# Adding the residual inside the mixing products' bank by TensorE transposes, instead of by kept copies and VectorE additions

## The chip, the cores and the metric

One core of a Trainium2 chip runs the whole program. The metric is the device time of one execution in microseconds (us). The kernel before takes 549.34 us (median of 3 runs, 549.34 to 549.35).

## The reference, cut to what matters

The program computes sparse attention, then a layer norm with a two-layer MLP (`x + relu(xn @ w_ch1) @ w_ch2`), and then a mixing block. The change is in the last one:

```
theta = x @ w_theta                           # x: (2, 768, 512)
zr, zi = x * cos(theta), x * sin(theta)
y = einsum('ts,bsd->btd', w_tok_r, zr) + einsum('ts,bsd->btd', w_tok_i, zi)
u = x + y
out = u + relu(u @ w_ch)
```

All values are float32. The products run on pairs: a value is split into a high part and a rest (`hi`, `lo`), and three products (hi*hi, hi*lo, lo*hi) stand for one.

## The kernel before, in words

The four working engines and SP each run their own list of instructions, written out in order; semaphores tie them together. Tokens are cut into 12 tiles of 128 (2 batches of 6), the 512 channels into 4 blocks of 128. `x` holds a token tile with tokens on partitions. The mixing wants its result the other way, channels on partitions (`y` transposed), so that the channel product can follow.

**Rotation.** For each token tile t (12 of them), `rotation_tensor` (L1313) first runs the 12 theta products of tile t-1 (L1323: 3 for each of 4 channel blocks, 512 columns) and then transposes tile t's four 128x128 blocks into `x2T_bank` (L1333). `rotation_scalar` (L1256) copies this bank to `x2Th` (L1261), then copies it a second time into a home that lasts (L1268, `x2T_home`, signal `x2T_kept`): two tiles have homes of their own, the others take the x tile of two tiles earlier, once its rotation is done (wait on `z_ready`). Then it computes abs and two sines for tile t-1 (L1276, L1277, L1279) and the high part of z for tile t-2 (L1284). `rotation_vector` (L1287) reduces theta to a fraction of a turn in three steps (L1295, L1297, L1299), subtracts for `x2Tl` (L1303), and makes `z_lo` (L1309). TensorE's next transposes wait for `x2T_split` and `x2T_kept`. GpSimd multiplies x by cosine and sine (L1232) and splits the token weights: SP loads a tile (L1190), GpSimd writes its high part (L1212) and its rest (L1215) into a ring of three slots, signal `tok_split`. A slot is free again once `ring_used` is raised, or, for the last tile of a group, once `y_mm` is. The last quarter of the MLP (L1087, L1105) runs between the first seven rotation steps.

**Mixing.** There are four groups n, one for each batch b and half th of the output tokens (384 columns). `mix(n)` in `mixing_tensor` runs over 6 input tiles s and 4 channel blocks d, with 6 products of 384 columns each (L1471), 144 in a group; each d has a PSUM bank of its own. In group 0, rotation steps 7 to 12 stand between its tiles. With the last s, each d raises `y_mm`. Then `u_add` (L1398) on VectorE adds the kept transposed x to the bank, in 3 pieces of 128 columns, into `u_sum`; ScalarE copies that to `uTh` (L1395); `u_low` subtracts for `uTl` (L1414). `channels(n)` (L1479) multiplies u by `w_ch` into the same banks (48 products, L1489), and runs one group late: the order on TensorE is mix 0, mix 1, channels 0, mix 2, channels 1, mix 3, channels 2, channels 3. `outputs(n)` on VectorE (L1424, L1428) forms u + relu, and SP stores it.

Of the kernel before, what the change touches and what calls it, by code (L numbers as in the profile page):

```python
# [20 lines left out]
F32 = mybir.dt.float32  # L21
# [66 lines left out]
def program(nc, qT, kcols, vwin, kT, v, limits, g_ln, w1, w2, w_theta, wtokT, w_ch, outT):  # L88
    with ExitStack() as ctx:
# [1053 lines left out]
        out_sb = placed("out_sb", 56, [P, 2, CN])  # L1143
        u_sum = placed("u_sum", 59, [P, 2, CN])

# [8 lines left out]
        c_hi, ch_hi, theta_split, ch_split, tok_split = sem("c_hi"), sem("ch_hi"), sem("theta_split"), sem("ch_split"), sem("tok_split")  # L1154
        x2T_mm, x2T_hi, x2T_split, x2T_kept = sem("x2T_mm"), sem("x2T_hi"), sem("x2T_split"), sem("x2T_kept")
        theta_mm, round_step, frac_ready, trig_ready = sem("theta_mm"), sem("round_step"), sem("frac_ready"), sem("trig_ready")
        abs_ready = sem("abs_ready")
        z_ready, z_high, z_split = sem("z_ready"), sem("z_high"), sem("z_split")
        ring_used, y_mm, u_added, u_high, u_split = sem("ring_used"), sem("y_mm"), sem("u_added"), sem("u_high"), sem("u_split")
        v_mm, u_summed, out_ready = sem("v_mm"), sem("u_summed"), sem("out_ready")  # L1160
        out_stored = [sem(f"out_stored{s}") for s in range(2)]

        MIX = [(b, th) for b in range(BATCH) for th in range(HALVES)]

        x2T_second = placed("x2T_second", 30, [P, DC, P])

        def x2T_home(t):

            if t == 0:
                return raw[:, 0, :, :].rearrange("p c n -> p (c n)")[:, DC * (FQ - P):].rearrange(  # L1170
                    "p (c n) -> p c n", c=DC)
            if t == 1:
                return x2T_second[:, :, :]
            return x_tile((t - AT) // TILES, (t - AT) % TILES)

# [32 lines left out]
        def mixing_pool(pool):  # L1208
# [8 lines left out]
            def split_tok(j):  # L1217
                pool.wait_ge(tok_loaded[j % 2], 16 * (j // 2 + 1))
                if j >= RING:
                    n, used = divmod(j - RING, TILES)  # L1220
                    if used == TILES - 1:
                        pool.wait_ge(y_mm, (n + 1) * DC)
                    else:
                        pool.wait_ge(ring_used, n * (TILES - 1) + used + 1)
                split(ring_h[j % RING][:, :, :], ring_l[j % RING][:, :, :], raw_tok[:, j % 2, :, :], tok_split)
# [30 lines left out]
        def rotation_scalar(act, t):  # L1256
            if t < TT:
                act.wait_ge(x2T_mm, t + 1)
                if t >= 2:
                    act.wait_ge(theta_mm, t - 1)  # L1260
                nc.scalar.activation(x2Th[:, t % 2, :, :].rearrange("p c n -> p (c n)"), x2T_bank[:, :],  # L1261
                                     ACT.Copy).then_inc(x2T_hi, 1)
                if t == 0:
                    act.wait_ge(theta_split, 1)
                elif t >= AT:
                    act.wait_ge(z_ready, t - AT + 1)
                act.wait_ge(x2T_split, t + 1)
                nc.scalar.activation(x2T_home(t), x2T_bank[:, :].rearrange("p (c n) -> p c n", c=DC),  # L1268
                                     ACT.Copy).then_inc(x2T_kept, 1)
            if 1 <= t < TT + 1:  # L1270
                m = t - 1
                s = m % 2
                act.wait_ge(frac_ready, m + 1)
                if m >= 2:
                    act.wait_ge(z_split, m - 1)
                nc.scalar.activation(frac[:, s, 1, :], frac[:, s, 0, :], ACT.Abs).then_inc(abs_ready, 1)  # L1276
                nc.scalar.activation(trig[:, s, 1, :], frac[:, s, 0, :], ACT.Sin, scale=TWO_PI)  # L1277
                act.wait_ge(abs_ready, m + 1)
                nc.scalar.activation(trig[:, s, 0, :], frac[:, s, 1, :], ACT.Sin, scale=-TWO_PI,  # L1279
                                     bias=half_pi[:, 0:1]).then_inc(trig_ready, 1)  # L1280
            if 2 <= t < TT + 2:
                m = t - 2
                act.wait_ge(z_ready, m + 1)
                nc.scalar.activation(z_hi[m // TILES][:, m % TILES, :, :], trig[:, m % 2, :, :],  # L1284
                                     ACT.Copy).then_inc(z_high, 1)
# [27 lines left out]
        def rotation_tensor(pe, t):  # L1313
# [12 lines left out]
            if t < TT:  # L1326

                pe.wait_ge(ch_added, CT * CHUNKS * LATE + t + 1)
                if t >= 1:
                    pe.wait_ge(x2T_split, t)  # L1330
                    pe.wait_ge(x2T_kept, t)
                for d in range(DC):
# [50 lines left out]
        def mixing_scalar(act):  # L1383
# [5 lines left out]
            for k in range(len(MIX) * DC):  # L1389
                th, d = MIX[k // DC][1], k % DC  # L1390
                act.wait_ge(u_added, CT * (k + 1))
                if k >= HALVES * DC:

                    act.wait_ge(out_ready, k - HALVES * DC + DC - d)
                nc.scalar.activation(uTh[:, th, d, :], u_sum[:, k % 2, :], ACT.Copy).then_inc(u_high, 1)  # L1395

        def mixing_vector(dve):
            def u_add(n, d):  # L1398

                b, th = MIX[n]  # L1400
                k = n * DC + d
                if k >= 2:
                    dve.wait_ge(u_split, k - 1)
                dve.wait_ge(y_mm, k + 1)
                for i in range(CT):
                    cols = slice(i * P, (i + 1) * P)
                    nc.vector.tensor_tensor(u_sum[:, k % 2, cols], mix_bank[th][d][:, cols],
                                            x2T_home(b * TILES + th * CT + i)[:, d, :], ALU.add).then_inc(u_added, 1)

            def u_low(n, d):  # L1410

                th, k = MIX[n][1], n * DC + d
                dve.wait_ge(u_high, k + 1)
                nc.vector.tensor_tensor(uTl[:, th, d, :], u_sum[:, k % 2, :],  # L1414
                                        uTh[:, th, d, :].bitcast(F32), ALU.subtract).then_inc(u_split, 1)

# [19 lines left out]
            for n in range(len(MIX)):  # L1436
                for d in range(DC + 1):
                    if d < DC:
                        u_add(n, d)
                    if d >= 1:  # L1440
                        u_low(n, d - 1)
                if n >= 1:
# [3 lines left out]
        def mixing_tensor(pe):  # L1446
            def mix(n):

                b, th = MIX[n]
                for s in range(TILES):  # L1450
# [5 lines left out]
                    for d in range(DC):  # L1456
# [7 lines left out]
                        if s == 0 and n == 1 and d == 0:  # L1464
                            pe.wait_ge(frac_ready, TT)
                            pe.wait_ge(x2T_kept, TT)
                        if s == 0 and n >= 2:
                            pe.wait_ge(out_ready, (n - 2) * DC + d + 1)
                        for r in range(2):
                            for m, (zt, wt) in enumerate(((z_hi, ring_h), (z_hi, ring_l), (z_lo, ring_h))):  # L1470
                                last = nc.tensor.matmul(bank, zt[b][:, s, r, ds], wt[j % RING][:, r, :],  # L1471
                                                        start=(s == 0 and r == 0 and m == 0),
                                                        stop=(s == TILES - 1 and r == 1 and m == 2))
                        if s == TILES - 1:
                            last.then_inc(y_mm, 1)
                    if s < TILES - 1:
# [88 lines left out]
```

## Time and profile before

| | |
|---|---|
| time, median of 3 | 549.34 us |
| profiled execution: its own time, and its span | 549.34 us, 547.5 us |
| PE (TensorE products) busy | 537.8 us (98%) |
| PEld (TensorE weight loads) busy | 482.0 us (88%) |
| DVE (VectorE) busy | 266.2 us (49%) |
| ACT (ScalarE) busy | 171.2 us (31%) |
| POOL (GpSimd) busy | 185.7 us (34%) |
| granted TensorE clock, mean | 1.00 |

Busy time is the union of an engine's instructions. Products overlap in the pipeline, so the record of a 384-column product is about twice as long as the distance from its start to the next one's: for a rate, starts are compared and not durations. The rotation runs from about 347 us on, the mixing from about 395 us to the end.

### The profile page before, as it was taken

The page shows a single profiled execution, that of the slowest core. Times are in us where ns is not written, and L with a number is a line of the kernel's source. Part 1 is how long each engine was busy: PE and PEld are TensorE (multiplying, and loading weights), DVE is VectorE, ACT ScalarE, POOL GpSimd, SP SyncE. Part 2 cuts the span into 40 slices and gives each one's busy share as a digit, 9 for nine tenths or more (in the row PEclk, how much of TensorE's full clock was granted, in tenths as well). Part 3 has the DMA queues.
Part 4 walks back from the last instruction along what each step waited for, and adds up shares of the span by engine and source line. Part 5 has one row for each costly group of instructions (what it writes and reads, how often), then busy time and mean ns, then how long its engine had stood idle before and what let it go on. Part 6 is the DMA issues. An engine that isn't in the chain of part 4 may idle for free.

```text
span 547.5 us, 8685 instructions
## 1 busy us (share of the span) xinstructions
PE 537.8 (98%) x3376; PEld 482.0 (88%) x3376; DVE 266.2 (49%) x678; ACT 171.2 (31%) x438; POOL 185.7 (34%) x165
## 2 busy tenths in 40 slices
PE   8899999999999999999999999999999999999997
PEld 7788788788888888998889998888799999999997
DVE  7765655556547454222222322355865669307054
ACT  5564443444435332111111111265555422001010
POOL 6596000000000000398000410033499799362500
PEclk9999999999999999999999999999999999999999
DMA  7663243211221000033100110000022133341202
GB/s 227 199 221 90 83 146 113 74 56 45 87 65 45 1 1 2 0 135 101 73 1 0 54 34 1 0 1 1 1 57 63 55 86 88 115 116 62 83 21 95
DMA packets 24810, 36.95 MB, mean 67 GB/s; under 512 B 2240, under 2 KB 17600, under 8 KB 24768
## 3 DMA queue, kind: packets, MB, share of 16 engines
q1 hardware_dynamic: 24768, 36.38, 21.4%
q8 instruction: 27, 0.44, 0.3%
q14 instruction: 15, 0.12, 0.1%
HBM read 33.23 MB, written 3.15 MB: 66 GB/s over the span
## 4 chain that ended last, share of the span: by engine, by line
PE 81%; POOL 10%; DVE 4%; issue 3%; ACT 1%; DMA 0%; POOLq 0%; DVEq 0%; ACTq 0%
PE bank L882 13%; PE bank L865 13%; PE bank L1471 12%; PE bank L1087 12%; PE bank L1105 11%; PE bank L1489 6%; POOL trig L1232 4%; PE bank L535 4%; PE bank L505 3%; PE bank L520 3%; POOL ring_l L1215 3%; PE bank L1323 3%; POOL ring_h L1212 2%; POOL bias L412 1%; PE bank L803 1%
## 5 line engine op out<-in xcount | busy, mean ns | idle before, releaser
L865 PE MATMUL bank<-xnT,w1h 128*128 128x256 f32 x384 | 73.7, 291 | 1.3 <-DVE xnT L826 1.3
L865 PEld LDWEIGHTS bank<-xnT,w1h 128*128 128x128 f32 x384 | 59.7, 191 | 7.2 <-issue 5.0
L1087 PE MATMUL bank<-xnT,w1h 128*128 128x384 f32 x256 | 65.2, 335 | 0.0
L1471 PE MATMUL bank<-ring_h,z_hi 128*128 128x384 f32 x192 | 65.0, 338 | 0.1
L1471 PE MATMUL bank<-ring_h,z_lo 128*128 128x384 f32 x192 | 64.3, 335 | 0.0
L1471 PE MATMUL bank<-ring_l,z_hi 128*128 128x384 f32 x192 | 64.2, 335 | 0.0
L484 ACT ACTIVATE sp_buf<-sp_buf,row_max 128x256 f32<-128x256 f32 (+1 forms) x96 | 46.0, 481 | 42.3 <-DVE row_max L428 42.3
L795 POOL TENSOR_TENSOR rstd<-rtmp,minus_half 128x2 f32<-128x2 f32 x6 | 4.2, 697 | 154.6 <-DVE rtmp L766 154.6
L1232 POOL TENSOR_TENSOR trig<-x,trig 128x512 f32<-128x512 f32 x24 | 32.8, 1387 | 67.7 <-ACT trig L1279 67.7
L865 PE MATMUL bank<-xnT,w1l 128*128 128x256 f32 x192 | 54.3, 283 | 0.0
L1215 POOL TENSOR_TENSOR ring_l<-raw,ring_h 128x768 fp32r<-128x768 f32 x24 | 48.0, 2001 | 2.0
L1087 PEld LDWEIGHTS bank<-xnT,w1h 128*128 128x128 f32 x256 | 46.4, 188 | 0.6
L1068 ACT ACTIVATE hTh<-bank 128x384 fp32r<-128x384 f32 x32 | 15.5, 490 | 99.4 <-PE bank L1087 99.4
L1087 PE MATMUL bank<-xnT,w1l 128*128 128x384 f32 x128 | 42.9, 335 | 0.0
L882 PE MATMUL bank<-w2h,hTh 128*128 128x512 f32 x96 | 40.8, 425 | 1.6 <-DVE hTl L845 1.3
L1048 DVE SCALAR_TENSOR_TENSOR hTl<-bank,hTh 128x384 fp32r<-128x384 f32 x32 | 17.7, 557 | 50.6 <-ACT hTh L1068 50.6
L1105 PE MATMUL bank<-w2h,hTh 128*128 128x512 f32 x96 | 38.0, 396 | 0.0
L882 PE MATMUL bank<-w2h,hTl 128*128 128x512 f32 x96 | 37.7, 393 | 0.0
L882 PE MATMUL bank<-w2l,hTh 128*128 128x512 f32 x96 | 37.7, 393 | 0.0
L1105 PE MATMUL bank<-w2h,hTl 128*128 128x512 f32 x96 | 37.6, 392 | 0.0
L428 DVE CUSTOM_DVE_ANT_0 sp_buf<-bank,bias 128x256 f32<-128x256 f32 (+1 forms) x96 | 32.9, 398 | 9.7 <-PE bank L505 7.7
L1105 PE MATMUL bank<-w2l,hTh 128*128 128x512 f32 x96 | 37.5, 391 | 0.0
(124 smaller groups left out, 1124.9 us busy)
## 6 DMA issues: line engine op xcount, KB each, us to landing
raw<-wtokT SPq DMA_DIRECT2D x24, 384.0 KB, 3.2
raw<-w SPq DMA_DIRECT2D x8, 1024.0 KB, 5.7
v_sb<-vwin SPq DMA_DIRECT2D x16, 256.0 KB, 2.7
k_sb<-kcols SPq DMA_DIRECT2D x16, 200.0 KB, 3.3
q_sb<-qT SPq DMA_DIRECT2D x24, 128.0 KB, 2.8
outT<-out_sb SPq DMA_DIRECT2D x16, 192.0 KB, 1.8
v_sb<-vwin SPq DMA_DIRECT2D x8, 192.0 KB, 2.9
k_sb<-kcols SPq DMA_DIRECT2D x8, 136.0 KB, 2.8
```

The source lines that it names most:

```text
L428: nc.vector.tensor_tensor_reduce(out=sp_buf[:, k % 2, u, h, 0:w], in0=score_banks(k)[h][:, u * WIN:u * WIN + w], in1=table_of[:, 2 * hp + ...
L484: nc.scalar.activation(scores, scores, ACT.Exp, scale=-1.0, bias=row_max[:, AT * k + u, h:h + 1], accum_out=den[:, AT * (k % DENS) + u, h, ...
L535: last = nc.tensor.matmul(o_bank(k)[DH * h:DH * (h + 1), u * P:(u + 1) * P], v_sb[:, s, value_chunk(t, u, c), DH * h:DH * (h + 1)], probsT ...
L865: last = nc.tensor.matmul(bank_of(n)[:, 0:AN], wt[q][:, d, f * P:(f + 1) * P], xnT[:, AT * c:AT * c + AT, low, d, :], start=(d == 0 and m ...
L882: last = nc.tensor.matmul(bank_of(n)[:, :], ht[:, f, i * P:(i + 1) * P], wt[q][:, f, :], start=(f == 0 and m == 0), stop=(f == FC - 1 and ...
L1048: nc.vector.scalar_tensor_tensor(hTl[:, f, :], h_bank[f % 2][:, 0:CN], 0.0, hTh[:, f, :].bitcast(F32), ALU.max, ALU.subtract).then_inc(h_s ...
L1087: last = nc.tensor.matmul(h_bank[f % 2][:, 0:CN], wt[slot][:, d, fs], tokens(low, d), start=first, stop=(d == DC - 1 and wt is w1l))
L1105: last = nc.tensor.matmul(ch_bank[i][:, :], ht[:, f, ts], wt[slot][:, f, :], start=(f == 0 and n == 0), stop=(f == FC - 1 and n == 2))
L1215: nc.gpsimd.tensor_tensor(lo, src, hi.bitcast(F32), ALU.subtract).then_inc(done, 1)
L1232: last = nc.gpsimd.tensor_tensor(tr, x_tile(t // TILES, t % TILES), tr, ALU.mult)
L1471: last = nc.tensor.matmul(bank, zt[b][:, s, r, ds], wt[j % RING][:, r, :], start=(s == 0 and r == 0 and m == 0), stop=(s == TILES - 1 and ...
L1489: last = nc.tensor.matmul(mix_bank[th][e][:, 0:CN], wt[:, d, es], ut[:, th, d, :], start=(d == 0 and m == 0), stop=(d == DC - 1 and m == 2))
```

## The change: the diff

The kept copies, their homes, `u_sum` and the additions go. When the last product of a bank in a mixing group is issued, three transposes (`is_transpose=True`, `start=False`) of the x blocks of those output tokens follow into the three 128-column pieces of the same bank; `y_mm` is raised behind the last one. ScalarE's `uTh` copy and VectorE's `uTl` subtraction read the bank. `ring_used` is now raised for each of a group's six tiles, for the sixth ahead of the last bank's transposes, and the ring's waits use it throughout.

```diff
--- before.py
+++ after.py
@@ -1141,7 +1141,6 @@
         ring_h = [placed(f"ring_h{s}", kb, [P, 2, CN], F32R) for s, kb in enumerate((24, 112, 118))]
         ring_l = [placed(f"ring_l{s}", kb + 3, [P, 2, CN], F32R) for s, kb in enumerate((24, 112, 118))]
         out_sb = placed("out_sb", 56, [P, 2, CN])
-        u_sum = placed("u_sum", 59, [P, 2, CN])
 
         x2T_bank, theta_bank = banks[0], (banks[1], banks[7])
         mix_bank = [banks[2:6], [banks[6], banks[7], banks[0], banks[1]]]
@@ -1152,26 +1151,15 @@
         theta_loaded, ch_loaded = sem("theta_loaded"), sem("ch_loaded")
         tok_loaded = [sem(f"tok_loaded{s}") for s in range(2)]
         c_hi, ch_hi, theta_split, ch_split, tok_split = sem("c_hi"), sem("ch_hi"), sem("theta_split"), sem("ch_split"), sem("tok_split")
-        x2T_mm, x2T_hi, x2T_split, x2T_kept = sem("x2T_mm"), sem("x2T_hi"), sem("x2T_split"), sem("x2T_kept")
+        x2T_mm, x2T_hi, x2T_split = sem("x2T_mm"), sem("x2T_hi"), sem("x2T_split")
         theta_mm, round_step, frac_ready, trig_ready = sem("theta_mm"), sem("round_step"), sem("frac_ready"), sem("trig_ready")
         abs_ready = sem("abs_ready")
         z_ready, z_high, z_split = sem("z_ready"), sem("z_high"), sem("z_split")
-        ring_used, y_mm, u_added, u_high, u_split = sem("ring_used"), sem("y_mm"), sem("u_added"), sem("u_high"), sem("u_split")
+        ring_used, y_mm, u_high, u_split = sem("ring_used"), sem("y_mm"), sem("u_high"), sem("u_split")
         v_mm, u_summed, out_ready = sem("v_mm"), sem("u_summed"), sem("out_ready")
         out_stored = [sem(f"out_stored{s}") for s in range(2)]
 
         MIX = [(b, th) for b in range(BATCH) for th in range(HALVES)]
-
-        x2T_second = placed("x2T_second", 30, [P, DC, P])
-
-        def x2T_home(t):
-
-            if t == 0:
-                return raw[:, 0, :, :].rearrange("p c n -> p (c n)")[:, DC * (FQ - P):].rearrange(
-                    "p (c n) -> p c n", c=DC)
-            if t == 1:
-                return x2T_second[:, :, :]
-            return x_tile((t - AT) // TILES, (t - AT) % TILES)
 
         def x_block(b, q, i):
             return x_tiles[:, b, i // AT, q, i % AT, :]
@@ -1217,11 +1205,7 @@
             def split_tok(j):
                 pool.wait_ge(tok_loaded[j % 2], 16 * (j // 2 + 1))
                 if j >= RING:
-                    n, used = divmod(j - RING, TILES)
-                    if used == TILES - 1:
-                        pool.wait_ge(y_mm, (n + 1) * DC)
-                    else:
-                        pool.wait_ge(ring_used, n * (TILES - 1) + used + 1)
+                    pool.wait_ge(ring_used, j - RING + 1)
                 split(ring_h[j % RING][:, :, :], ring_l[j % RING][:, :, :], raw_tok[:, j % 2, :, :], tok_split)
 
             def rotate(t):
@@ -1260,13 +1244,6 @@
                     act.wait_ge(theta_mm, t - 1)
                 nc.scalar.activation(x2Th[:, t % 2, :, :].rearrange("p c n -> p (c n)"), x2T_bank[:, :],
                                      ACT.Copy).then_inc(x2T_hi, 1)
-                if t == 0:
-                    act.wait_ge(theta_split, 1)
-                elif t >= AT:
-                    act.wait_ge(z_ready, t - AT + 1)
-                act.wait_ge(x2T_split, t + 1)
-                nc.scalar.activation(x2T_home(t), x2T_bank[:, :].rearrange("p (c n) -> p c n", c=DC),
-                                     ACT.Copy).then_inc(x2T_kept, 1)
             if 1 <= t < TT + 1:
                 m = t - 1
                 s = m % 2
@@ -1328,7 +1305,6 @@
                 pe.wait_ge(ch_added, CT * CHUNKS * LATE + t + 1)
                 if t >= 1:
                     pe.wait_ge(x2T_split, t)
-                    pe.wait_ge(x2T_kept, t)
                 for d in range(DC):
                     last = nc.tensor.transpose(x2T_bank[:, d * P:(d + 1) * P], x_block(t // TILES, d, t % TILES),
                                                ident[:, :])
@@ -1388,31 +1364,19 @@
             nc.scalar.activation(wch[:, :, :], raw_ch, ACT.Copy).then_inc(ch_hi, 1)
             for k in range(len(MIX) * DC):
                 th, d = MIX[k // DC][1], k % DC
-                act.wait_ge(u_added, CT * (k + 1))
+                act.wait_ge(y_mm, k + 1)
                 if k >= HALVES * DC:
 
                     act.wait_ge(out_ready, k - HALVES * DC + DC - d)
-                nc.scalar.activation(uTh[:, th, d, :], u_sum[:, k % 2, :], ACT.Copy).then_inc(u_high, 1)
+                nc.scalar.activation(uTh[:, th, d, :], mix_bank[th][d][:, 0:CN], ACT.Copy).then_inc(u_high, 1)
 
         def mixing_vector(dve):
-            def u_add(n, d):
-
-                b, th = MIX[n]
-                k = n * DC + d
-                if k >= 2:
-                    dve.wait_ge(u_split, k - 1)
-                dve.wait_ge(y_mm, k + 1)
-                for i in range(CT):
-                    cols = slice(i * P, (i + 1) * P)
-                    nc.vector.tensor_tensor(u_sum[:, k % 2, cols], mix_bank[th][d][:, cols],
-                                            x2T_home(b * TILES + th * CT + i)[:, d, :], ALU.add).then_inc(u_added, 1)
-
-            def u_low(n, d):
-
-                th, k = MIX[n][1], n * DC + d
-                dve.wait_ge(u_high, k + 1)
-                nc.vector.tensor_tensor(uTl[:, th, d, :], u_sum[:, k % 2, :],
-                                        uTh[:, th, d, :].bitcast(F32), ALU.subtract).then_inc(u_split, 1)
+            def u_low(n):
+                th = MIX[n][1]
+                for d in range(DC):
+                    dve.wait_ge(u_high, n * DC + d + 1)
+                    nc.vector.tensor_tensor(uTl[:, th, d, :], mix_bank[th][d][:, 0:CN],
+                                            uTh[:, th, d, :].bitcast(F32), ALU.subtract).then_inc(u_split, 1)
 
             def outputs(n):
                 th = MIX[n][1]
@@ -1434,11 +1398,7 @@
             nc.vector.tensor_tensor(wcl[:, :, :], raw_ch, wch[:, :, :].bitcast(F32),
                                     ALU.subtract).then_inc(ch_split, 1)
             for n in range(len(MIX)):
-                for d in range(DC + 1):
-                    if d < DC:
-                        u_add(n, d)
-                    if d >= 1:
-                        u_low(n, d - 1)
+                u_low(n)
                 if n >= 1:
                     outputs(n - 1)
             outputs(len(MIX) - 1)
@@ -1463,15 +1423,19 @@
                                 pe.wait_ge(ch_added, CT * CHUNKS * LATES - CT + d - 1)
                         if s == 0 and n == 1 and d == 0:
                             pe.wait_ge(frac_ready, TT)
-                            pe.wait_ge(x2T_kept, TT)
                         if s == 0 and n >= 2:
                             pe.wait_ge(out_ready, (n - 2) * DC + d + 1)
                         for r in range(2):
                             for m, (zt, wt) in enumerate(((z_hi, ring_h), (z_hi, ring_l), (z_lo, ring_h))):
                                 last = nc.tensor.matmul(bank, zt[b][:, s, r, ds], wt[j % RING][:, r, :],
-                                                        start=(s == 0 and r == 0 and m == 0),
-                                                        stop=(s == TILES - 1 and r == 1 and m == 2))
+                                                        start=(s == 0 and r == 0 and m == 0), stop=False)
                         if s == TILES - 1:
+                            if d == DC - 1:
+                                last.then_inc(ring_used, 1)
+                            for i in range(CT):
+                                last = nc.tensor.matmul(bank[:, i * P:(i + 1) * P], x_block(b, d, th * CT + i),
+                                                        ident[:, :], start=False, stop=(i == CT - 1),
+                                                        is_transpose=True)
                             last.then_inc(y_mm, 1)
                     if s < TILES - 1:
                         last.then_inc(ring_used, 1)
```

## Rows read from the trace of the kernel before

**Rows 1.** The page, the chain that ended last, by engine

```profile
PE 81%; POOL 10%; DVE 4%; issue 3%; ACT 1%; DMA 0%; POOLq 0%; DVEq 0%; ACTq 0%
```

**Rows 2.** Chain of waits, pieces from 442 us: start us, us, what

```profile
442.37 1.85 POOL ring_l L1215
...
444.26 17.08 PE bank L1471 x96
...
502.94 24.96 PE bank L1471 x144
527.90 16.66 PE bank L1489 x96
```

**Rows 3.** Busy by stretch: length, PE, PEld, DVE, ACT, POOL, clock, DMA share, GB/s

```profile
347.00:391.70 44.70, 43.79 (x215) 36.70 (x214) 24.13 (x36) 22.90 (x38) 13.08 (x10) 1.00 0.00 1
391.70:444.30 52.60, 52.46 (x285) 48.86 (x285) 34.43 (x35) 26.28 (x40) 45.56 (x31) 1.00 0.19 53
444.30:545.00 100.70, 100.25 (x576) 99.74 (x576) 46.39 (x98) 10.33 (x17) 45.52 (x30) 1.00 0.27 85
```

**Rows 4.** Instruction groups of PE, 391.7 to 443.8: busy, mean ns, idle

```profile
L1471 PE MATMUL bank<-ring_h,z_hi 128*128 128x384 f32 x64 | 21.9, 342 | 0.0
...
L1323 PE MATMUL bank<-wth,x2Tl 128*128 128x512 f32 x24 | 9.5, 394 | 0.0
...
L1333 PE MATMUL bank<-ident,x 128*128 128x128 f32 x20 | 3.0, 273 | 0.0
```

**Rows 5.** One line's instructions (L1333), then PE's timeline: start, us, what

```profile
L1333 PE MATMUL bank<-ident,x x48: 272/273/273, 347.6 to 424.4; 128*128 128x128 f32 x48
...
424.07 0.60 PE L1333 MATMUL bank<-ident,x 128*128 128x128 f32 x4
424.43 0.42 PE L1471 MATMUL bank<-ring_h,z_hi 128*128 128x384 f32 x1
424.69 0.33 PE L1471 MATMUL bank<-ring_l,z_hi 128*128 128x384 f32 x1
```

**Rows 6.** PE's timeline, earlier short products, and line L505's records

```profile
23.78 0.95 PE L893 MATMUL bank<-ident 128*128 128x128 f32 x7
...
41.80 1.04 PE L520 MATMUL bank<-ident,sp_buf 128*128 128x128 f32 x8
...
60.44 1.14 PE L535 MATMUL bank<-probsT,v_sb 128*64 128x128 f32 x16
...
L505 PE MATMUL bank<-k_sb,q_sb x192: 271/377/632, 4.8 to 191.0; 64*128 64x256 f32 x160, 64*128 64x128 f32 x32
```

**Rows 7.** The kept copy, L1268: its records, and who waited (no line follows)

```profile
L1268 ACT ACTIVATE x<-bank x10: 597/599/602, 362.3 to 427.3; 128x512 f32<-128x512 f32 x10
...
who waited for it (us, times):
```

**Rows 8.** PE's timeline at one theta step, and ahead of 444 us

```profile
384.92 0.40 PE L1105 MATMUL bank<-w2h,hTl 128*128 128x512 f32 x1
385.74 0.47 PE L1323 MATMUL bank<-wth,x2Th 128*128 128x512 f32 x1 [0.42 <-DVE x2Tl L1303]
...
443.79 0.34 PE L1471 MATMUL bank<-ring_h,z_lo 128*128 128x384 f32 x1
```

**Rows 9.** Timelines of DVE and POOL

```profile
384.91 0.68 DVE L1303 TENSOR_TENSOR x2Tl<-bank,x2Th 128x512 fp32r<-128x512 f32 x1
...
394.63 2.73 POOL L1232 TENSOR_TENSOR trig<-x,trig 128x512 f32<-128x512 f32 x2 [3.25 <-ACT trig L1279]
...
431.55 2.73 POOL L1232 TENSOR_TENSOR trig<-x,trig 128x512 f32<-128x512 f32 x2 [3.02 <-ACT trig L1279]
```

**Rows 10.** Instruction groups, 372 to 548 us: busy, mean ns, idle before

```profile
L1414 DVE TENSOR_TENSOR uTl<-u_sum,uTh 128x384 fp32r<-128x384 f32 x16 | 14.5, 918 | 0.3
...
L1407 DVE TENSOR_TENSOR u_sum<-bank,x 128x128 f32<-128x128 f32 x40 | 9.4, 284 | 42.2 <-PE bank L1471 42.0
L1395 ACT ACTIVATE uTh<-u_sum 128x384 fp32r<-128x384 f32 x16 | 8.4, 526 | 73.9 <-DVE u_sum L1407 73.8
```

## The prediction

> **What bounds the kernel now.** I read the chain of waits first: 81% of it is TensorE, 10% GpSimd [rows 1]. The change touches the last third of the program, so I followed that chain from 442 us: at 444.26 it leaves GpSimd's ring split for TensorE, and from there to 544.56 it is nothing but L1471 and L1489, back to back, with one DVE add and the store behind them [rows 2]. Then the busy times by stretch: after 444.3 TensorE is busy 100.25 of 100.70 us, and its weight loads 99.74, at clock 1.00; DVE, ACT and GpSimd have half or more of the stretch free. From 391.7 to 444.3 TensorE has 52.46 of 52.60 us, and before it 43.79 of 44.70 [rows 3].
>
> Modelled busy time can hide waiting, and the chain between 388 and 444 us runs over GpSimd, so I checked the second stretch by start-to-start distances. L1471 takes 24.96 us for 144 products, 0.173 us each [rows 2]. L1323 has 512 columns instead of 384 and starts every 0.23 us (0.173 x 512/384 = 0.231, my estimate); a transpose starts every 0.11 us, as shown below. The stretch from 391.70 to 443.8 holds 3 x 64 products of L1471, 3 x 24 of L1323 and 20 transposes [rows 4]: 192 x 0.173 + 72 x 0.23 + 20 x 0.11 = 33.2 + 16.6 + 2.2 = 52.0 us of the 52.3 that passed. So TensorE really runs without a gap there too, and GpSimd keeps pace beside it. The bound is TensorE's instruction count from about 391 us to the end.
>
> **What the change adds on TensorE.** For each of 4 (batch, half) groups and 4 banks, three transposes of 128 columns are put in front of the y_mm signal: 4 x 4 x 3 = 48. Their x block is the loaded weight and ident streams, as in L1333, of which the trace has 48 records for the 12 x 4 that the code issues, so one record each [rows 5]. The price by L1333: a group of four starts at 424.07 and has 0.60 us from first start to last end, the last lasting 0.273, so three distances in 0.327 us, 0.109 each; and the second product behind it starts at 424.69, where without the group it would have started at 424.07 + 0.173: 0.62 - 0.173 = 0.447 us for four, 0.112 each, the switch to fp32 and back included [rows 5]. Eight of L520 give the same 0.109 ((1.04 - 0.275)/7) [rows 6]. A 128-column stream costs that much although 384 columns take 0.173: each transpose needs its own weights, and the next load starts only as the previous stream begins. The load ahead of the first transpose hides under the product before it, the load for the product behind the last one does not, so I take three as 3 x 0.11. Sum: 48 x 0.11 = 5.28 us.
>
> Bounds for one such accumulating transpose, which the trace does not show (all the ones it has overwrite their columns): from below L535, 128 columns with a half-wide weight, (1.14 - 0.28)/15 = 0.057 us, 2.7 us in all; from above an ordinary fp32 product, which leaves two records (L505: 192 for the 24 x 4 that the code issues), and whose records start every (0.95 - 0.275)/6 = 0.1125 us at L893 [rows 6]: 0.225 us, 10.8 us in all. I take L1333's 0.11: it is the same instruction on the same operands apart from the accumulate flag, and products in this trace that accumulate go at the rate of their columns.
>
> The trace's price for a lone stream can be set against the Trainium skill, "TensorE: Matmul & The Clock Gate", section "Back-to-back issue gap", which gives about 81 ns per load-and-product pair at 128 columns once sustained. By that figure the 48 would be an estimated 3.9 us. The trace's rows give 0.109 to 0.112, and I stay with them.
>
> All 48 are in program order on TensorE. The 12 at the end of the first mixing group fall at about 435.6 us, the other 36 in the stretch that the chain follows to the end. No engine's slack covers them, with one exception. At 443.79 the last product ahead of the ninth ring tile starts and the next at 444.26, 0.47 instead of 0.173 us [rows 8, 2]: TensorE waits 0.30 us for GpSimd's ring_l, which ends at 444.22. The first 12 transposes bring TensorE there 1.32 us later, and GpSimd does not move (its split waits on a ring slot freed before the transposes). So that 0.30 us goes: 5.28 - 0.30 = **+4.98 us**. What is late next is TensorE itself. If GpSimd were also 1.3 us later there, the 0.30 would stay: +5.28.
>
> **What the change takes from DVE and ACT in the mixing.** 48 additions of 0.28 us on DVE (40, 4 and 4 in three groups) go; the ACT copy and the DVE subtraction stay and read a bank instead of u_sum [rows 10]. Worth nothing: ACT sat idle 73.8 us for these copies, and the products that want u_split start a whole mixing group later, except in the last group, where the 8.3 us of channels(2) (half of the 16.66 at 527.90 [rows 2]) stand before channels(3). The banks are held until the subtraction ends, which channels(n) waited for before. If reading the bank made the subtraction slower (0.918 us mean now [rows 10]), even 2 us for each of the four would just fill those 8.3 us. The last add and the store are unchanged.
>
> **What it takes from the rotation.** 12 ACT copies of 0.60 us go, with the waits before them and TensorE's x2T_kept wait; nobody in the trace waited for these copies, TensorE included [rows 7]. What ACT sat idle ahead of them it sits idle later, at abs, for z_lo. The two real stalls of TensorE there are another's: theta's first product starts at 385.74, 0.82 us after the product before instead of 0.23 (0.59 lost; 0.62 again at 391.70), released by x2Tl [rows 8]. x2Tl runs at 384.91, right behind DVE's own three frac steps, which start when the previous theta ends [rows 9]; no ACT copy stands in that chain. Value taken: 0. The end above: ACT's relief somehow removes both, -1.21. The end below: earlier sines let GpSimd rotate beside DVE more often and delay x2Tl once more, +0.6. The re-aimed ring waits (ring_used for y_mm) free a slot at the same product as before: 0.
>
> **Sum.** Against the profiled execution's own 549.34 us (span 547.5 and 1.84 around it): 549.34 + 4.98 = **554.3 us**. The median of the three runs is the same 549.34, so nothing is to be shifted. +0.91%.
>
> **Rivals.**
> (a) Cheaper transposes or freed stalls: 48 x 0.057 = 2.7 less 0.3 gives 551.8; price 0.11 with both theta stalls gone gives 549.34 + 4.98 - 1.21 = 553.1. For it: only one of the three loads needs to hide. Against: two families of transposes at 0.109. Chance 0.09.
> (b) The accumulating transpose does not get the short form and runs as an ordinary fp32 product, so the change doesn't do what it says: 48 x 0.225 - 0.3 = +10.5, 559.8 us. For it: no such instruction is in the trace. Against: the same transpose flag as L1333's. Chance 0.07.
> (c) Not slower: GpSimd, not TensorE, paces 388 to 444 us, as the chain says. Then what it waited for ACT's sines counts, 3.25 us at 394.63 and 3.02 at 431.55 [rows 9], and with ACT rid of its copies and of the z_ready wait these 6.27 us come back, with the 0.30: 5.28 - 6.57 = -1.3, 548.0 us. It decides from the point at which TensorE's 52.3 us hold more than 5 us of waiting. Against it: my count leaves 0.3 us. Chance 0.03, with 0.01 for stopping within 0.2%.
> (d) The granted clock falls to 1.2 GHz over the new groups. In the rows it is 1.00 over all twelve groups of L1333 [rows 3]. Half rate over a bank's last six products and its three transposes (6 x 0.173 + 0.33 = 1.37 us) would add 1.37 us, 16 times: 549.34 + 4.98 + 21.9 = 576 us. Chance 0.01.
> What (d) goes by is the same page of the Trainium skill, section "Part 4: PE-mode transpose", which says that transposes do not count as activity for the clock gate. The trace shows no fall behind groups of four or eight, so it bears the rule out at no place that matters here.
>
> **Chances.** Forecast 0.79; (a) 0.09, (b) 0.07, (c) 0.04, (d) 0.01. Range 552.2 to 556.0: below, most of (a); above, the missing 0.30, the 0.6 of a new stall and 0.01 us more for each transpose. Outside are (b), (c), (d) and the bottom of (a), some 0.15. A difference under 0.2% (1.1 us) can't be told from none here. Faster 0.03, same 0.01, slower 0.96.
>
> **What would show it.** The new transpose line: 48 records, starts 0.11 us apart; 0.22 and 96 records mean (b). Each mixing group from 444 us on 1.3 us longer, 26.3 instead of 24.96; channels still 8.32. The wait for ring_l at the ninth tile gone; theta's stalls still two, released by x2Tl. Clock 1.00 throughout. DVE's and ACT's busy time down by about 14 and 7 us, with no effect on the end. The forecast is wrong if the mixing groups keep 24.96 us, or if 391 to 444 us shrinks by more than 1 us.

## The result, and the profile after

The changed kernel takes 554.49 us (median of 4 runs, 554.33 to 554.70), the kernel before 549.34 us beside it: ratio 1.0094, interval 1.0077 to 1.0112. It is slower, by 5.15 us. The forecast was 554.3 us and +0.91%. The profiled execution took 554.20 us, 4.86 more than the profiled one of before; the sum of the prediction said 4.98.

The page of the changed kernel, its shares of the chain (compare [rows 1]):

```profile
PE 92%; DVE 4%; POOL 1%; issue 1%; ACT 1%; DMA 0%; DVEq 0%; POOLq 0%; ACTq 0%
```

GpSimd's 10% are down to 1%. GpSimd did not get faster: TensorE's wait for it at 444 us is gone, and with it the way by which the chain used to step over to GpSimd's list for 55 us. A share of the chain says where the walk back went, and 0.3 us of waiting can decide that.

The chain of waits from 471 us to the end (start us, us, what; compare [rows 2]):

```profile
471.80 21.85 PE bank L1430 x126
493.65 0.33 PE bank L1436 x3
493.98 1.05 PE bank L1430 x6
...
497.79 0.33 PE bank L1436 x3
498.12 8.33 PE bank L1453 x48
506.44 21.85 PE bank L1430 x126
...
532.76 16.66 PE bank L1453 x96
```

L1430 is the mixing product (L1471 before), L1436 the new transpose, L1453 the channel product (L1489 before). A mixing group runs from 471.80 to 498.12, 26.32 us instead of 24.96; the channel products keep 8.33 and 16.66.

Busy times by stretch, columns as in [rows 3], up to the last rotation product, then up to the first, second and third block of channel products:

```profile
391.72:431.48 39.76, 39.76 (x213) 36.48 (x213) 27.02 (x29) 17.96 (x29) 32.98 (x22) 1.00 0.22 60
431.48:463.23 31.75, 31.75 (x193) 31.45 (x192) 14.77 (x14) 9.67 (x15) 28.79 (x18) 1.00 0.26 75
463.23:497.87 34.64, 34.64 (x207) 34.49 (x206) 7.84 (x12) 1.97 (x4) 16.10 (x12) 1.00 0.30 92
497.87:532.51 34.64, 34.64 (x207) 34.49 (x206) 7.85 (x12) 1.97 (x4) 10.71 (x8) 1.00 0.18 57
```

TensorE is busy all of each, at clock 1.00. The first stretch took 39.76 us before as well, with ACT busy 21.54 instead of 17.96: the missing copies show on ACT and nowhere in time. Two rows for it and the second stretch, of the kernel before:

```profile
391.70:431.46 39.76, 39.76 (x213) 36.47 (x213) 26.98 (x29) 21.54 (x35) 32.98 (x22) 1.00 0.21 60
431.46:461.18 29.72, 29.58 (x169) 29.08 (x168) 21.08 (x34) 9.81 (x14) 28.37 (x17) 1.00 0.26 72
```

The second one grew by 2.03 us, with 24 transposes in it; the third and fourth, 33.28 us each before (by the chain, 24.96 + 8.32), by 1.36 us with 12 each.

The new line's records, and TensorE's timeline around the first group of three (compare [rows 5]):

```profile
L1436 PE MATMUL bank<-ident,x x48: 270/272/273, 432.5 to 532.5; 128*128 128x128 f32 x48
```

```profile
432.36 0.34 PE L1430 MATMUL bank<-ring_h,z_lo 128*128 128x384 f32 x1
432.54 0.49 PE L1436 MATMUL bank<-ident,x 128*128 128x128 f32 x3
432.78 0.42 PE L1430 MATMUL bank<-ring_h,z_hi 128*128 128x384 f32 x1
433.04 0.34 PE L1430 MATMUL bank<-ring_l,z_hi 128*128 128x384 f32 x1
```

48 records, so the short form. From 432.36 to 433.04 there are 0.68 us, 0.35 of them for the two long products: 0.33 for three transposes. Three starts span 0.49 - 0.272 = 0.218 us, 0.109 apart, and the rest falls on the next product, which is followed after 0.26 us instead of 0.173.

### The profile page after: what moved, and what is told of

It is laid out like the page before. It is cut to its first block, busy times and chain, and to the rows that moved or that the text cites. A ratio compares the mean times of both kernels' runs of the same rounds, so it can differ in the third digit from the quotient of the medians.

```text
span 552.4 us, 8695 instructions
## 1 busy us (share of the span) xinstructions
PE 542.3 (98%) x3424; PEld 486.5 (88%) x3424; DVE 250.4 (45%) x630; ACT 163.7 (30%) x426; POOL 183.2 (33%) x165
## 4 chain that ended last, share of the span: by engine, by line
PE 92%; DVE 4%; POOL 1%; issue 1%; ACT 1%; DMA 0%; DVEq 0%; POOLq 0%; ACTq 0%
PE bank L1430 18%; PE bank L882 13%; PE bank L865 13%; PE bank L1087 12%; PE bank L1105 11%; PE bank L1300 6%; PE bank L1453 6%; PE bank L535 4%; PE bank L505 3%; PE bank L520 3%; POOL bias L412 1%; PE bank L1436 1%; PE bank L1309 1%; PE bank L803 1%; PE bank L545 1%
## 5 line engine op out<-in xcount | busy, mean ns | idle before, releaser
L1430 PE MATMUL bank<-ring_h,z_hi 128*128 128x384 f32 x192 | 65.9, 343 | 0.0
L1430 PE MATMUL bank<-ring_h,z_lo 128*128 128x384 f32 x192 | 64.4, 336 | 0.0
L1430 PE MATMUL bank<-ring_l,z_hi 128*128 128x384 f32 x192 | 64.3, 335 | 0.0
L1203 POOL TENSOR_TENSOR ring_l<-raw,ring_h 128x768 fp32r<-128x768 f32 x24 | 46.8, 1951 | 2.0
L1200 POOL TENSOR_SCALAR ring_h<-raw 128x768 fp32r<-128x768 f32 x24 | 25.2, 1050 | 36.9 <-DMA raw<-wtokT 25.3
```

The source lines that it names most:

```text
L1200: nc.gpsimd.tensor_scalar(hi, src, 1.0, 0.0, ALU.mult, ALU.add).then_inc(c_hi, 1)
L1203: nc.gpsimd.tensor_tensor(lo, src, hi.bitcast(F32), ALU.subtract).then_inc(done, 1)
```

## The experiments

The edits are cut to the lines that matter. In e1, e3, e4 and e6 the ring's waits are also those of the kernel before.

The theory under test: TensorE's list is the bound, each transpose costs 0.11 us wherever it stands, what left DVE and ACT was free, and the one thing gained is the wait for the ninth ring tile (`ring_l`, the rest of a token weight tile that GpSimd splits).

**e1: the removals alone.** The 48 transposes are left out, so the residual is not added.

```diff
-                            for i in range(CT):
-                                last = nc.tensor.matmul(bank[:, i * P:(i + 1) * P], x_block(...), ident[:, :], ...)
                             last.then_inc(y_mm, 1)
```

> The changed kernel with its 48 transposes left out, so the residual is not added to u; the ring waits are those of before. All that the change removes is gone, and what it adds too. Theory (the removed copies and additions are worth nothing, TensorE's instruction count is the bound): 549.3 us, with the wait for ring_l at the ninth tile back. Rival (the relief of ACT, DVE or GpSimd is worth something, and the transposes cost more than 5.1 us): 548.1 us or less.

Measured: 549.41 us (median of 10, 549.29 at best), ratio to before 1.0002 (0.9992 to 1.0012). Its chain:

```profile
442.33 1.86 POOL ring_l L1203
...
444.24 17.07 PE bank L1434 x96
...
527.87 16.66 PE bank L1451 x96
```

The same pieces as in [rows 2], to 0.04 us. 48 DVE additions, 12 ACT copies and their waits are worth nothing, and the wait for ring_l is back. So all of the 5.15 us lies in the transposes. The re-aimed ring waits, which e1 does not have, show no effect either: e3 and e4 have the transposes with the old ring waits and come within 0.2 us of the changed kernel.

**e2: the transpose as an ordinary product.**

```diff
-                                                        is_transpose=True)
+                                                        )
```

> The changed kernel with the transpose flag dropped: the same x block times the same identity as an ordinary fp32 product, into the same columns. Theory (it leaves two records, each with a weight load of its own, at 0.112 us): 96 records, another 48 x 0.112 = 5.4 us, so 559.9 us. Rival (one pass with a longer stream, or a slower stream only): under 557 us.

Measured: 559.78 us, 5.3 us above the changed kernel. Its records of the line, loads and products:

```profile
L1436 PEld LDWEIGHTS bank<-ident,x x96: 187/192/192, 434.0 to 539.4; 128*128 128x128 f32 x96
L1436 PE MATMUL bank<-ident,x x96: 271/275/275, 434.1 to 539.5; 128*128 128x128 f32 x96
```

Twice the records, at 5.3 / 48 = 0.11 us for each one more: rival (b) has this price. It did not happen: with the flag an adding transpose leaves one record, 48 in the changed kernel.

**e3: transposes one by one between long products.**

```diff
                                 last = nc.tensor.matmul(bank, zt[b][:, s, r, ds], wt[j % RING][:, r, :], ...)
+                                if s == TILES - 1 and r == 0:
+                                    nc.tensor.matmul(bank[:, m * P:(m + 1) * P], x_block(b, d, th * CT + m),
+                                                     ident[:, :], start=False, stop=False, is_transpose=True)
```

> The changed kernel with the three transposes of a bank set singly between the last tile's products, one behind each of the first three. Theory (what a transpose costs is the load of the next weights, which cannot start before its own stream does, wherever it stands): 0.11 us each again, or up to 0.14 as each now pays for the switch back to a 384-column product: 554.5 to 555.6 us. Rival (in a row the short streams starve the loads, between long ones they hide; then a transpose costs its 128 columns, 0.058 us by 0.173 x 128 / 384): 549.3 + 2.8 - 0.3 = 551.9 us.

Measured: 554.32 us, ratio to before 1.0085 (1.0068 to 1.0102), 0.2 under the lower end of what was expected. TensorE's timeline:

```profile
431.62 0.27 PE L1438 MATMUL bank<-ident,x 128*128 128x128 f32 x1
431.65 0.42 PE L1434 MATMUL bank<-ring_l,z_hi 128*128 128x384 f32 x1
431.91 0.27 PE L1438 MATMUL bank<-ident,x 128*128 128x128 f32 x1
431.93 0.42 PE L1434 MATMUL bank<-ring_h,z_lo 128*128 128x384 f32 x1
432.19 0.27 PE L1438 MATMUL bank<-ident,x 128*128 128x128 f32 x1
```

One transpose and one long product take 431.91 - 431.62 = 0.29 us, 0.28 at the next pair: 0.11 to 0.12 on top of 0.173. Singly between long products they cost what they cost three in a row, so this interleaving did not make them cheap; others were not tried. That the weight load is the cause is what the distances fit: at L535 [rows 6] the same 128 streamed columns with a weight half as wide start 0.057 us apart, no more than 128 columns of a long product take (0.173 / 3 = 0.058), so the stream's own width does not make the 0.11 us. But L535 differs in more than that width, and no run changed the load alone: the load as the cause is argued, the 0.11 us is shown.

**e4: the transposes ahead of the products, overwriting.**

```diff
+                        if s == 0:
+                            for i in range(CT):
+                                nc.tensor.matmul(bank[:, i * P:(i + 1) * P], x_block(b, d, th * CT + i),
+                                                 ident[:, :], start=(i == 0), stop=False, is_transpose=True)
```

The three behind the last product go, and the first product adds instead of overwriting.

> The changed kernel with the three transposes ahead of a bank's first product instead of behind its last, the first of them overwriting the bank, the products adding to them. Theory (adding costs no more than overwriting, and place does not matter while TensorE is the bound): 554.4 us, starts 0.11 us apart. The ninth ring tile's wait is hidden by now 24 transposes ahead of it instead of 12. Rival (adding into a bank costs extra, 0.03 us of each transpose): 553.0 us. Second rival (groups 2 and 3 start with a wait for out_ready, and the transposes' place there moves that wait or the first groups' start): over 555 us.

Measured: 554.44 us (554.16 at best), within 0.1 us of the changed kernel. The first of each three carries the start flag, and all three stand in a bank that holds no sums yet. Adding into a bank has no price of its own that these runs can tell. The second rival is out too: in the trace the third group's transposes follow channels(0) without a gap.

**e5: each transpose twice** (the residual is added twice).

```diff
-                            for i in range(CT):
+                            for k, i in enumerate(list(range(CT)) * 2):
```

> The changed kernel with each of the three transposes issued twice, so that the residual is added twice: 96 instead of 48. Theory (each transpose costs the same 0.11 us, nothing of the first 48 was hidden beyond the ring wait): another 48 x 0.11 = 5.3 us, 559.7 us; six in a row span 5 x 0.109 + 0.273 = 0.82 us from first start to last end. Rival (part of the first 48 was covered by slack, so that the second 48 cost more than the first 5.1 us): over 560.5 us.

Measured: 559.57 us, 5.08 us for the second 48, 0.106 each. The first 48 had cost 5.15 us, net of the waits that they hid (the executions of one kernel differ by 0.2 to 0.4 us, so the medians tell no more than that the two are alike). The timeline:

```profile
434.03 0.34 PE L1430 MATMUL bank<-ring_h,z_lo 128*128 128x384 f32 x1
434.20 0.82 PE L1436 MATMUL bank<-ident,x 128*128 128x128 f32 x6
434.78 0.42 PE L1430 MATMUL bank<-ring_h,z_hi 128*128 128x384 f32 x1
435.04 0.33 PE L1430 MATMUL bank<-ring_l,z_hi 128*128 128x384 f32 x1
```

Six cost 435.04 - 434.03 - 0.35 = 0.66 us, 0.11 each, and span the expected 0.82 us.

**e6: no transposes in the first mixing group** (its residual is not added).

```diff
-                            for i in range(CT):
+                            for i in range(CT if n else 0):
```

> The changed kernel with the transposes of the first mixing group left out (its residual is not added): 36 of 48. Theory (the first group's 12 hide the wait for ring_l, the other 36 cost in full): the wait at the ninth ring tile comes back, 0.3 to 0.6 us, and 12 x 0.113 = 1.36 us go: 553.4 to 553.7 us. Rival (the wait went because of something else, as the freed ACT and DVE, and stays gone): 553.1 us, and no wait for ring_l in the chain.

Measured: 553.67 us. Twelve transposes less (1.36 us by the other groups) brought 0.82, so some 0.54 us came back elsewhere. TensorE's timeline says where:

```profile
444.14 0.34 PE L1434 MATMUL bank<-ring_h,z_lo 128*128 128x384 f32 x1
444.65 0.44 PE L1434 MATMUL bank<-ring_h,z_hi 128*128 128x384 f32 x1 [0.17 <-POOL ring_l L1203]
```

From 444.14 to 444.65 are 0.51 us instead of 0.173: the wait is back, with everything that relieved DVE and ACT still in place. It is the first group's 12 transposes that cover it, and not the relief of any engine.

**e9: the kernel before, with the ninth ring tile split ahead of the last rotation.**

```diff
-            for t in range(TILES, TT):
+            for t in range(TILES, TT - 1):
                 rotate(t)
                 split_tok(j)
                 j += 1
+            split_tok(j)
+            rotate(TT - 1)
+            j += 1
```

> The kernel before, with one change on GpSimd: the ninth ring tile is split ahead of the last tile's rotation instead of behind it. Theory: the ring wait goes, 0.3 to 0.6 us, 548.8 to 549.0 us, TensorE without a gap from 391 us to the end. Rival (the later rotation makes z_lo, wch and the first u late, and channels(0) waits): 549.4 us or more.

Measured: 548.81 us, ratio to before 0.9984 (0.9975 to 0.9992), as expected. It is the fastest version of this study, by 0.5 us only. Its chain has no wait from 431 us on:

```profile
431.64 29.14 PE bank L1474 x168
460.79 8.32 PE bank L1492 x48
469.11 24.96 PE bank L1474 x144
```

The last rotation is needed by the third group's last tile, at about 490 us (469.11 + 5/6 x 24.96), the ring tile at once; the order on GpSimd had it the other way round. The rival (channels(0) waits for the later u) did not come.

**e7: the kernel before, with x2Tl ahead of the frac steps at rotation steps 5 and 6.**

```diff
 def rotation_vector(dve, t):
+    if t in (5, 6):
+        x2_low()                      # the x2Tl subtraction
     if 1 <= t < TT + 1: ...           # frac, three steps
-    if t < TT:
+    if t < TT and t not in (5, 6):
         x2_low()
```

> The kernel before, with one change on DVE: at rotation steps 5 and 6 x2Tl is made ahead of the three frac steps instead of behind them. TensorE's two theta stalls (0.59 and 0.62 us) should go. Theory (behind them the ninth ring tile's rest on GpSimd is the next bound, already 0.30 us late): the 1.2 us come back as a longer wait for ring_l, 549.3 us. Rival (TensorE alone is the bound): 548.1 us.

Measured: 549.28 us, as the theory said, and for another reason. Timeline of ACT (abs, z_hi, then x2Th; the two sines stand between the first and the second), and of TensorE:

```profile
387.61 0.63 ACT L1276 ACTIVATE frac<-frac 128x512 f32<-128x512 f32 x1 [2.32 <-DVE z_lo L1313]
...
389.28 1.04 ACT L1284 ACTIVATE z_hi<-trig 128x1024 fp32r<-128x1024 f32 x1
390.23 0.57 ACT L1261 ACTIVATE x2Th<-bank 128x512 fp32r<-128x512 f32 x1
```

```profile
384.93 0.40 PE L1105 MATMUL bank<-w2h,hTl 128*128 128x512 f32 x1
385.17 0.39 PE L1327 MATMUL bank<-wth,x2Th 128*128 128x512 f32 x1
...
390.19 0.40 PE L1105 MATMUL bank<-w2h,hTl 128*128 128x512 f32 x1
391.68 0.47 PE L1327 MATMUL bank<-wth,x2Th 128*128 128x512 f32 x1 [1.09 <-DVE x2Tl L1290]
```

The first stall is gone (384.93 to 385.17, a plain 0.24). The second grew from 0.62 to 1.26 us: with frac later, z_lo is later, ACT's abs and sines with it, and the next step's x2Th stands behind them on ACT. TensorE is back on its old time there (391.70 in the kernel before) and never reaches the ring with the gain. Then it loses another 0.30 us ahead of the theta products at 399.4, behind an x2Tl that ends at 399.28, and 0.13 us at 402.7, behind a ring_l that ends at 402.68 (the second ring tile). So it comes to the ninth ring tile some 0.45 us later than in the kernel before, GpSimd is 0.2 us earlier there, and the tile is ready: its 168 mixing products from 432.09 us take 29.14 us, as in e9. The theory wanted a longer wait for ring_l there; there is none.

**e8 and e10: the same edit on e9, and on the changed kernel.**

> The kernel before with both edits, x2Tl ahead at steps 5 and 6, and the ninth ring tile ahead of the last rotation. Theory (two waits in series, each hiding the other's gain): 549.34 - 1.21 - 0.3 to 0.6 = 547.5 to 547.8 us, faster than both kernels. Rival: 549.0 us, a third wait takes their place (ring_l of an earlier tile, or u_split).

> The changed kernel with x2Tl ahead at steps 5 and 6. Theory (the first group's 12 transposes already give GpSimd 1.36 us, of which the ring wait used 0.3 to 0.6): the 1.21 us of the theta stalls come back but for 0.15 to 0.45 us: 553.3 to 553.7 us. Rival (nothing comes back): 554.4 us.

Measured: 549.29 us and 554.62 us. Both theories missed; e8 lies above its rival too, and e10 at its rival (nothing comes back). The edits of e8 and e10 on DVE are e7's, and e10's timeline has e7's stall:

```profile
390.18 0.40 PE L1105 MATMUL bank<-w2h,hTl 128*128 128x512 f32 x1
391.67 0.47 PE L1304 MATMUL bank<-wth,x2Th 128*128 128x512 f32 x1 [1.09 <-DVE x2Tl L1267]
```

Behind it come e7's other two, 0.3 us ahead of the theta products at 399.4 and 0.12 to 0.13 us at 402.8, in e8 and e10 alike. In e8 that is 1.68 us of waiting, where e9 keeps its 1.19, and the 0.49 us between them are the 0.48 by which e8 is slower than e9. And e8 takes e7's time, 549.29 against 549.28: the ring wait that its second edit removes was already gone in e7.

**e11: e9's edit, x2Tl ahead at steps 5 to 7, and x2Th of steps 6 and 7 ahead of z_hi on ACT.** Of the edit, only the part on ACT:

```diff
+            if t + 1 in (6, 7):
+                x2_high(t + 1)        # the x2Th copy, taken from the head of the next step
             if 2 <= t < TT + 2: ...   # z_hi
```

> The kernel before with the ninth ring tile ahead of the last rotation, x2Tl ahead of the frac steps on DVE at rotation steps 5, 6 and 7, and on ACT x2Th of steps 6 and 7 ahead of z_hi. Theory (with x2Tl alone ahead, the second stall grew to 1.26 us because x2Th(6) stood behind the later sines and z_hi; without z_hi in front it is ready 0.96 us earlier): the stalls shrink from 1.19 us to about 0.3 us, 548.81 - 0.9 = 547.9 us. Rival (DVE's and ACT's own chain of frac, z_lo, abs and sines is simply as long as TensorE's step, so the delay only moves on to steps 7 and 8): 548.6 us or more.

Measured: 549.37 us, where the rival said 548.6 or more. The two stalls did shrink, to one of 0.31 us. But rotations and sines slipped later (abs starts at 394.29 us, at 392.78 in the kernel before), and the second ring tile's rest on GpSimd with them; TensorE waited for it 1.1 us. So the delay moved on as the rival has it, and is paid at the ring:

```profile
399.73 2.76 POOL L1215 TENSOR_TENSOR ring_l<-raw,ring_h 128x768 fp32r<-128x768 f32 x1
```

```profile
400.99 0.60 PE L1346 MATMUL bank<-ident,x 128*128 128x128 f32 x4
402.54 0.44 PE L1484 MATMUL bank<-ring_h,z_hi 128*128 128x384 f32 x1 [0.95 <-POOL ring_l L1215]
```

## Why the prediction was right, point by point

**The bound.** Right. Counting starts against elapsed time gave 0.3 us of waiting between 391 and 444 us although the chain ran over GpSimd there. e1 settles it: DVE and ACT relieved, nothing gained. Rival (c) is out by more than 6 us.

**48 transposes at 0.11, 5.28 us.** Right within 3%. By the chain the third and fourth group grew by 1.36 us each, with no wait in them before or after. The first two had waits before, so e9 is the measure: its 168 products of that stretch take 29.14 us without a gap, and the changed kernel's 168 with 24 transposes take 31.84 (431.64 to 463.48), 2.70 more. Taken as 4 x 1.36 it is 5.44 in all, 0.113 a transpose. L1333's distance was the right row: the accumulate flag does not change it (e4), nor does standing singly (e3), and the next 48 cost the same (e5). The nearest rows were better than the general figure: the 81 ns for a pair in the Trainium skill, "TensorE: Matmul & The Clock Gate", section "Back-to-back issue gap", would have given an estimated 3.9 us, and 5.4 was measured.

**The ring wait, -0.30.** Right in kind and place (e6, e9), half in size. The first two groups grew by 2.03 us up to the start of the first channel product, and by 2.12 to the start of the second, since the first one, right behind three transposes, is followed after 0.26 us instead of 0.173. 2 x 1.36 is 2.72, so 0.60 us of waiting went. Of that, 0.30 is the wait. The product behind it took another 0.11 us more than its 0.173 before it let the next one start, and I had not counted that. And I missed a second wait of the same kind, 0.14 us, two tiles later. These are 0.55 of the 0.60 us; e6 got 0.54 back, and e9 gained 0.53. Both rows of the kernel before:

```profile
444.26 0.44 PE L1471 MATMUL bank<-ring_h,z_hi 128*128 128x384 f32 x1
444.54 0.34 PE L1471 MATMUL bank<-ring_l,z_hi 128*128 128x384 f32 x1
...
452.54 0.34 PE L1471 MATMUL bank<-ring_h,z_lo 128*128 128x384 f32 x1
452.75 0.45 PE L1471 MATMUL bank<-ring_h,z_hi 128*128 128x384 f32 x1
453.03 0.34 PE L1471 MATMUL bank<-ring_l,z_hi 128*128 128x384 f32 x1
```

444.26 to 444.54 is 0.28 us; 452.54 to 453.03 is 0.49 for two products that take 0.35. GpSimd's ring_l of that tile ran from 450.85 for 1.85 us, to 452.70. The two errors, 0.16 us too little for the transposes and 0.30 too little for the waits, go against each other, and that the sum came within 0.12 us of the profile is in part luck: 5.44 - 0.60 = 4.84 us, with the 0.02 by which the mixing began later 4.86, as the profile has it; the forecast said 5.28 - 0.30 = 4.98.

**DVE's and ACT's work in the mixing, 0.** Right. DVE's subtraction even became faster, and ACT's copy a little; neither is seen in the time:

```profile
L1378 DVE TENSOR_TENSOR uTl<-bank,uTh 128x384 fp32r<-128x384 f32 x16 | 8.6, 554 | 59.5 <-ACT uTh L1371 59.5
L1371 ACT ACTIVATE uTh<-bank 128x384 fp32r<-128x384 f32 x16 | 7.5, 491 | 78.6 <-PE bank L1436 78.6
```

**The rotation, 0.** Right: the stalls at 385.7 and 391.7 stand in the changed kernel too (0.59 and 0.60 us). The lower of the two ends that I kept (both stalls gone) did not come even on purpose: e7, e8 and e10 removed the first stall and e11 all but 0.31 us of both, and each time the gain was lost at a later wait.

**The clock.** 1.00 in every stretch with transposes, also with six in a row (e5). What the Trainium skill says of transposes, that a transpose "doesn't count as PE-busy the same way" ("TensorE: Matmul & The Clock Gate", section "Part 4: PE-mode transpose"), made no difference here, with a third of a microsecond of transposes in each 1.4 at the end of a group.

## What to carry to other kernels

Where one engine's list is the bound, work given to it has its full price, less the waits that it covers, and here the relief of the others was worth nothing, however long they were busy: 16 us less on DVE (266.2 to 250.4) and 7.5 less on ACT (171.2 to 163.7) against 5.4 us of TensorE made the kernel 5.15 us slower. Price a short product by the distance between starts of its like in the trace (0.11 us here) and not by its columns (0.058 us). A stall's worth is what is left at the next wait: before counting it, ask what the edit that removes it makes late.

## What the runs showed of the hardware that was not expected

A 128x384 subtraction on DVE took 0.918 us on the mean from SBUF [rows 10] and 0.554 from a PSUM bank (the row above). In the kernel before, the slow ones lie where GpSimd runs its splits (1.86 us at 451.25), the others take 0.55; in the changed kernel none is slow, though they run beside the same splits. What makes the difference was not isolated.

e4's profiled execution took 556.14 us where its others took 554.16 to 554.47. Its row for 25 to 30 us, and e3's:

```profile
25.00:30.00 5.00, 3.31 (x19) 2.93 (x19) 3.25 (x10) 2.56 (x8) 3.84 (x5) 0.80 0.29 78
```

```profile
25.00:30.00 5.00, 3.53 (x28) 3.02 (x28) 2.93 (x10) 2.89 (x9) 4.17 (x5) 1.00 0.35 98
```

The clock is down to 0.80 on the mean of those 5 us, with 19 products done instead of 28, and TensorE was idle for about a third of the stretch in both. It is far from the change. The profiled executions of e2 and e5 (561.23 us each, 1.4 to 1.8 above their others) have the same 0.80 in this stretch, and their timelines above run 1.5 to 1.7 us later than the changed kernel's; e6's has the same 3.31 us of work in the stretch as e4's and keeps 1.00. What set the clock off in some executions and not in others, the runs don't show.
